# A feed-forward of two layers: plain products against Strassen's seven, through DRAM

## The chip, the cores and the metric

The kernel runs on one core of a Trainium2 chip. The metric is the device time of one execution in microseconds. A core has TensorE (PE in the profile; its weight loads are PEld), VectorE (DVE), ScalarE (ACT), GpSimd (POOL) and SyncE (SP, which here only issues DMAs), each with its own queue that runs in order. SBUF is the on-chip memory of 128 partitions; matmuls write PSUM, 8 banks of 512 fp32 columns.

## The reference

```python
def reference(q, k, v, moe_w_in, moe_w_out, moe2_w_in, moe2_w_out):
    # 4 batches, 8 heads, 576 tokens, head size 64; causal window of 128, a bias by distance
    scores = where(mask, q @ k.T / sqrt(64) + bias, -1e9)
    attn_out = softmax(scores) @ v
    x = attn_out.transpose(0, 2, 1, 3).reshape(2304, 512)
    h = x @ moe_w_in                               # 512 -> 2048
    x = (h * sigmoid(1.702 * h)) @ moe_w_out       # 2048 -> 512
    h = x @ moe2_w_in
    g = where(h >= 1, h, where(h <= -1, 0, (h + 1) ** 2 / 4))
    return g @ moe2_w_out
```

## The kernel before

Attention comes first (`attend` on each engine): 32 heads in 4 batches, 5 blocks of queries a head, software-pipelined by fixed lags. Its result stands transposed in `x_all` (features on partitions, all 2304 tokens).

Then two feed-forward layers, each over 6 chunks of 384 tokens (`feed_forward`, loops over chunks are hardware loops from chunk 1 on). To keep fp32 precision at one pass a column, each operand is split in two parts: `hi` is the value rounded to fp32r (ScalarE copies), `lo` is the value less `hi` (a VectorE subtraction), and a product is three matmuls: hi·hi, hi·lo, lo·hi. For each of 16 tiles j of 128 hidden features, `up` runs 12 matmuls of 384 columns (4 feature tiles x 3) into one of 4 PSUM banks. ScalarE applies the activation out of PSUM (layer 1: one Gelu_apprx_sigmoid; layer 2: `activate` with two Relu, `clip` on VectorE, `square` on ScalarE, a sum on VectorE), VectorE rounds and splits it (`split_activations`), and `down`, two tiles behind, adds it into 4 accumulator banks (layer 1: 4 x 3 matmuls of 384 columns, weights stationary, result transposed) or 3 (layer 2: 3 x 3 matmuls of 512 columns, activations stationary, result in rows of tokens). The 16 weight tiles of a layer (512 KB each) come by DMA through the ring `w_raw` of 3, are rounded and split once in the first chunk (`round_weights`, `split_weights`) and stay in SBUF. A chunk's result goes back into `x_all`, in layer 2 from there to `out`.

While attention ends, `FIRST_UPS` puts the first three `up` of 12 matmuls between its last steps on TensorE, and GpSimd splits the first three weight tiles and the first chunk of x.

All order is written out by hand: each engine's program text is its order, and semaphores tie the engines.

## Time and profile before

| | us |
|---|---|
| median of 3 runs | 973.02 (972.94 to 973.79) |
| the profiled execution | 972.23 |
| its span, first to last instruction | 970.4 |

| slices 1 to 40, tenths busy | |
|---|---|
| PE | 5999999999999999999999999999999999999998 |
| DVE | 6777774653213223232232277644444544544543 |
| ACT | 4777787332112121111121166543443533434433 |
| POOL | 3666574000000000000000000000000000000000 |
| DMA | 9966850430000000000000034010100100100101 |

The span is cut in 40 equal slices of 24 us; a digit is the busy share in tenths. Attention is the first 7 slices, layer 1 runs to slice 23, layer 2 to the end. A matmul's record overlaps the next one's, since matmuls are pipelined: their pace is read from starts, or from the chain, and not from the mean duration of one. The granted clock is 0.999 over the span.

### The profile page before, as it was taken

To read this page: it belongs to the slowest core of one execution; us is meant where nothing else is said; L and a number is where in the kernel's file an instruction comes from. 1 tells how busy PE (TensorE), PEld (TensorE's weight loads), DVE (VectorE), ACT (ScalarE), POOL (GpSimd) and SP (SyncE) were. 2 spreads that over 40 slices of the span, in tenths; PEclk is the share of its full clock that TensorE was granted. 3 is DMA by queue.
4 is the path that set the end of the run, shared out by engine and by line. 5 is a ranking of instruction groups with operands and counts; after the bars stand their busy time and mean duration, and the time that the engine had idled before them with its cause. 6 is when DMAs were issued, how large, how long until landed. Compare 5 with 4: busy or idle time off the path is not lost.

```text
span 970.4 us, 16335 instructions
## 1 busy us (share of the span) xinstructions
PE 955.9 (99%) x5584; PEld 903.1 (93%) x5584; DVE 443.4 (46%) x1156; ACT 377.9 (39%) x907; POOL 96.0 (10%) x71
## 2 busy tenths in 40 slices
PE   5999999999999999999999999999999999999998
PEld 5999999999999999999999999899999999998997
DVE  6777774653213223232232277644444544544543
ACT  4777787332112111121121166543443433534433
POOL 3666574000000000000000000000000000000000
PEclk9999999999999999999999999999999999999999
DMA  9966850430000000000000034010100100100101
GB/s 228 228 163 157 221 130 28 131 130 22 1 1 0 0 0 0 0 0 0 0 0 0 0 131 133 20 33 1 33 0 0 32 0 0 32 0 0 32 0 32
DMA packets 27729, 46.62 MB, mean 48 GB/s; under 512 B 5040, under 2 KB 19504, under 8 KB 27696
## 3 DMA queue, kind: packets, MB, share of 16 engines
q1 hardware_dynamic: 27696, 46.21, 18.0%
q8 instruction: 17, 0.28, 0.1%
q14 instruction: 16, 0.13, 0.1%
HBM read 41.48 MB, written 4.72 MB: 48 GB/s over the span
## 4 chain that ended last, share of the span: by engine, by line
PE 98%; DMA 1%; SPq 0%; DVE 0%; issue 0%; ACT 0%; DVEq 0%
PE bank L463 41%; PE bank L409 41%; PE bank L370 7%; PE bank L334 5%; PE bank L351 3%; PE bank L383 1%; DMA qk_raw<-qkT 1%; PE bank L390 0%; SPq L230 0%; DVE qk_hi L638 0%; DVE qk_hi L644 0%; ACT x_all L573 0%; SPq L258 0%; SPq L259 0%; DVE probs L657 0%
## 5 line engine op out<-in xcount | busy, mean ns | idle before, releaser
L586 ACT ACTIVATE act_a<-bank 128x384 f32<-128x384 f32 x96 | 47.1, 490 | 306.4 <-PE bank L409 306.4
L409 PE MATMUL bank<-x_hi,w_hi_b 128*128 128x384 f32 x480 | 161.6, 337 | 0.0
L409 PE MATMUL bank<-x_hi,w_lo_b 128*128 128x384 f32 x480 | 161.5, 336 | 0.0
L409 PE MATMUL bank<-x_lo,w_hi_b 128*128 128x384 f32 x480 | 161.3, 336 | 0.0
L713 DVE CAST g_hi<-act_a 128x384 fp32r<-128x384 f32 x96 | 34.5, 359 | 266.3 <-PE bank L463 251.0
L589 ACT ACTIVATE act_a<-bank,halves 128x384 f32<-128x384 f32 x96 | 55.6, 579 | 193.2 <-PE bank L409 193.2
L409 PE MATMUL bank<-x_hi,w_hi_a 128*128 128x384 f32 x288 | 97.2, 337 | 0.0
L409 PE MATMUL bank<-x_hi,w_lo_a 128*128 128x384 f32 x288 | 96.9, 336 | 0.0
L409 PE MATMUL bank<-x_lo,w_hi_a 128*128 128x384 f32 x288 | 96.8, 336 | 0.0
L409 PEld LDWEIGHTS bank<-x_hi,w_hi_b 128*128 128x128 f32 x480 | 90.2, 188 | 2.8
L409 PEld LDWEIGHTS bank<-x_lo,w_hi_b 128*128 128x128 f32 x480 | 90.3, 188 | 2.7
L409 PEld LDWEIGHTS bank<-x_hi,w_lo_b 128*128 128x128 f32 x480 | 90.3, 188 | 0.0
L753 DVE TENSOR_SCALAR act_a<-act_a 128x384 f32<-128x384 f32 x96 | 34.5, 360 | 118.4 <-ACT act_a L589 118.4
L708 DVE TENSOR_TENSOR act_r<-act_a,act_r 128x384 f32<-128x384 f32 x96 | 53.6, 558 | 63.4 <-ACT act_a L596 63.4
L463 PE MATMUL bank<-g_hi,w_lo_b 128*128 128x384 f32 x240 | 80.7, 336 | 0.0
L463 PE MATMUL bank<-g_lo,w_hi_b 128*128 128x384 f32 x240 | 80.7, 336 | 0.0
L463 PE MATMUL bank<-g_hi,w_hi_b 128*128 128x384 f32 x240 | 80.7, 336 | 0.0
L505 ACT ACTIVATE probs<-probs,neg_max 128x256 f32<-128x256 f32 (+2 forms) x160 | 74.3, 467 | 15.2 <-DVE neg_max L657 13.5
L370 PE MATMUL bank<-v_sb,probs_t 128*128 128x64 f32 (+2 forms) x576 | 76.0, 263 | 0.1
L370 PEld LDWEIGHTS bank<-v_sb,probs_t 128*128 128x128 f32 (+2 forms) x576 | 67.2, 178 | 5.7 <-issue 0.5
L463 PE MATMUL bank<-w_hi_b,g_lo 128*128 128x512 f32 x180 | 71.0, 394 | 0.0
L463 PE MATMUL bank<-w_lo_b,g_hi 128*128 128x512 f32 x180 | 70.9, 394 | 0.0
(75 smaller groups left out, 1856.4 us busy)
## 6 DMA issues: line engine op xcount, KB each, us to landing
qk_raw<-qkT SPq DMA_DIRECT2D x64, 288.0 KB, 4.6
w_raw<-w_tiles SPq DMA_DIRECT2D x32, 512.0 KB, 3.3
out<-x_all SPq DMA_DIRECT2D x18, 256.0 KB, 2.7
v_sb<-v_main SPq DMA_DIRECT2D x32, 128.0 KB, 4.1
bias_sb<-bias_table SPq DMA_DIRECT2D x8, 128.0 KB, 5.8
v_sb<-v_tail SPq DMA_DIRECT2D x32, 16.0 KB, 3.9
ident<-identity SPq DMA_DIRECT2D x1, 64.0 KB, 3.9
```

Source lines behind the costliest of these rows:

```text
L334: last = nc.tensor.matmul(score_bank[n % SCORE_RING][0:rows, 0:BAND], qk_hi[:, slot, 0, blk * P:blk * P + rows], k[:, key0:key0 + BAND], s ...
L351: last = nc.tensor.transpose(pt_bank[half][0:keys, col:col + rows], probs[0:rows, n % PROB_RING, piece * P:piece * P + keys], ident[0:rows ...
L370: last = nc.tensor.matmul(o_bank[0:rows, blk * DIM:(blk + 1) * DIM], probs_t[0:keys, half, col:col + rows], v_sb[0:keys, h, key_tile], sta ...
L383: last = nc.tensor.transpose(xt_bank[:, blk * P:(blk + 1) * P], heads_out[:, blk, pair * P:(pair + 1) * P], ident[:])
L409: last = nc.tensor.matmul(hid_bank[j % HID_RING][:, 0:CHUNK], w(j)[:, 0, k * P:(k + 1) * P], x[:, k], start=n_mm == 0, stop=n_mm == 3 * KT ...
L463: last = nc.tensor.matmul(to, stationary, moving, start=j == 0 and n_pass == 0, stop=j == FT - 1 and n_pass == 2)
L505: nc.scalar.activation(at, at, ACT.Exp, bias=neg_max[0:rows, n % PROB_RING:n % PROB_RING + 1], scale=-1.0, accum_out=sums[0:rows, h % SUM_ ...
L586: nc.scalar.activation(act_a[:, s], hidden, ACT.Gelu_apprx_sigmoid).then_inc(act_ready, 1)
L589: nc.scalar.activation(act_a[:, s], hidden, ACT.Relu, bias=halves[:, 0:1], scale=0.5).then_inc(act_first, 1)
L708: nc.vector.tensor_tensor(act_r[:, s], act_a[:, s], act_r[:, s], ALU.add).then_inc(act_summed, 1)
L713: nc.vector.tensor_copy(g_hi[:, s], g[:, s]).then_inc(g_rounded, 1)
L753: nc.vector.tensor_scalar(act_a[:, s], act_a[:, s], 1.0, None, ALU.min).then_inc(act_clipped, 1)
```

## The change

Strassen's algorithm multiplies two matrices, each cut in 2 x 2 quadrants, with 7 products of quadrants for 8 (in Winograd's form here). The left operand's sums are S1 = A21 + A22, S2 = S1 - A11, S3 = A11 - A21, S4 = A12 - S2; the weights get three chained sums for each tile (`add_weights`: 2 quadrants at once, 1, 1). The products are P1 (A11), P5 (S1), P6 (S2), P2 (A12), P7 (S3), P3 (S4), P4 (A22), in this order, and TensorE adds them in PSUM onto copies ("seeds") of partial sums: C11 = P1 + P2; P6 goes onto P1; C12, C21 and C22 are built from that with D1 = P5.

The work: 4 phases u (layer u // 2, half of the hidden features u % 2). A phase is up over 3 chunks of 768 tokens, then down over 3 chunks; these are the 8 phases of the title line, 4 up and 4 down. A chunk is two halves of 384 tokens by two halves of the features. A "duo" D is two hidden tiles in each half at once: an up chunk has two duos, a down chunk one. A product of a duo has two halves (`pos`), each of 6 matmuls of 384 columns in up, 12 of 384 in down of layer 1, and in down of layer 2 36 matmuls of 256 columns for both.

The other engines, for each chunk k and each duo D (all in the order of `up` and `down` on each queue):
- `round_operand` (ScalarE) and `split_operand` (VectorE) for each of the 7 operands, 768 columns in up and 1536 in down; `sum_operand` (VectorE) for S1 to S4.
- `seed_b` twice, `copy_d` twice, `seed_c` (ScalarE, out of PSUM; seeds also into PSUM); C11 and C21 by ScalarE, C22 and C12 by VectorE. In phases of odd u the down results are added to a partial result that is loaded back (`load_partial`, `add_c11`, `add_c21`).
- The activation: layer 1 Gelu_apprx_sigmoid on C11 and C21 out of PSUM and on 1536 columns in SBUF; layer 2 a clip to [-1, 1] of 3072 columns (VectorE), a square with bias and scale (ScalarE) and a maximum with g (VectorE), 3072 columns each.
- Weights: 8 tiles a phase of 512 KB, through one staging buffer `wst`, which is loaded again only when the tile before is split. In up, tiles w2 and w3 are prepared in chunk 0, w4 and w5 in chunk 1, w6 and w7 in chunk 2; w0 and w1 of the next phase in the first two down chunks.

Through DRAM go x (`store_pair`, `load_x`), the hidden activations (`store_hidden`, 1.57 MB a duo; `load_hidden`, four loads of 0.79 MB a down chunk) and the results of every phase (`store_y`). All are issued on SyncE's queue in one fixed order, each behind its waits. All loops of the feed-forward are unrolled. In attention, the pairs of heads go to `x_pairs` instead of `x_all`, and ScalarE, VectorE and GpSimd prepare two weight tiles and four operands in the last batch; `FIRST_PRODUCTS` puts three product halves (18 matmuls) and two marks between the last attention steps.

The core of the diff:

```diff
-CHUNK = 384
+HALF = 384
+CHUNK = 2 * HALF
...
+PHASES = 4
+DUOS = 9
+OPS = 7
+P1, P5, P6, P2, P7, P3, P4 = range(OPS)
+A11, S1, S2, A12, S3, S4, A22 = range(OPS)
...
+        def multiply(u, up, k, D, i, pos, bank, start):
+            at = operand(k, i)
+            dd = D % DUOS % 2
+            if up:
+                w = w_op(8 * u + 2 * dd + pos, i)
+                steps = [(bank, w[:, wh, kt * P:(kt + 1) * P], at[:, xh, kt])
+                         for kt in range(2) for wh, xh in ((0, 0), (0, 1), (1, 0))]
+            elif u < 2:
+                steps = [(bank, w_op(8 * u + 4 + kt, i)[:, wh, pos * P:(pos + 1) * P], at[:, xh, kt])
+                         for kt in range(4) for wh, xh in ((0, 0), (0, 1), (1, 0))]
+            else:
+                steps = [(bank[:, n * 2 * P:(n + 1) * 2 * P], at[:, xh, kt, (2 * pos + n) * P:(2 * pos + n + 1) * P],
+                          w_op(8 * u + 4 + kt, i)[:, wh])
+                         for n in range(2 - pos) for kt in range(4) for wh, xh in ((0, 0), (1, 0), (0, 1))]
...
+        def product_6(u, up, c, k, D, n):
+            pe.wait_ge(lo_made, OPS * k + S2 + 1)
+            pe.wait_ge(seeded_b, 2 * D + n + 1)
...
+        def product_4(u, up, c, k, D, n):
+            pe.wait_ge(lo_made, OPS * k + A22 + 1)
+            pe.wait_ge(c22_done, D + 1)
```

From ScalarE's `up`:

```diff
+        def up(u, c):
+            k = up_chunk(u, c)
+            D = up_duo(u, c, 0)
+            seed_b(D, 0)
+            round_operand(k, S3)
+            seed_b(D, 1)
+            round_operand(k, S4)
+            copy_d(D, 0)
+            if c:
+                activate(u, c - 1, 1)
+            if c == 0:
+                round_weights(8 * u + 2)
+            seed_c(D)
+            copy_d(D, 1)
+            round_operand(k, A22)
+            up_c11(u, c, 0)
+            if c == 0:
+                round_weights(8 * u + 3)
+            if c == 1:
+                round_weights(8 * u + 4)
+            up_c21(u, c, 0)
+            D = up_duo(u, c, 1)
+            seed_b(D, 0)
+            if c < 2:
+                round_operand(k + 1, A11)
+            seed_b(D, 1)
+            copy_d(D, 0)
+            activate(u, c, 0)
+            if c == 2:
+                round_weights(8 * u + 6)
+            seed_c(D)
+            copy_d(D, 1)
+            if c == 2:
+                round_operand(k + 1, A11)
+            round_operand(k + 1, S1)
+            up_c11(u, c, 1)
```

From VectorE's `up` (k is the up chunk, u the phase, c the chunk in it), and from SyncE:

```diff
+            sum_operand(k, S3)
+            sum_operand(k, S4)
+            if u >= 2 and c:
+                clip(u, c - 1, 1)
+            if c == 0:
+                add_all_weights(8 * u + 2)
+            split_operand(k, S3)
+            split_operand(k, S4)
+            if c == 0:
+                split_weights(8 * u + 2)
+            if u >= 2 and c:
+                larger(u, c - 1, 1)
+            split_operand(k, A22)
+            if c == 0:
+                add_all_weights(8 * u + 3)
+            if c == 1:
+                add_all_weights(8 * u + 4)
+            if c == 2:
+                add_all_weights(8 * u + 6)
+            up_c22(u, c, 0)
...
+            up_c12(u, c, 0)
+            if u >= 2:
+                clip(u, c, 0)
+            sum_operand(k + 1, S1)
+            if c == 2:
+                split_weights(8 * u + 6)
+            split_operand(k + 1, A11)
+            if u >= 2:
+                larger(u, c, 0)
+            split_operand(k + 1, S1)
+            sum_operand(k + 1, S2)
+            if c == 1:
+                add_all_weights(8 * u + 5)
+            if c == 2:
+                add_all_weights(8 * u + 7)
+            up_c22(u, c, 1)
...
+        def load_weights(w):
+            wait_past(sp, w_ready, 2 * w)
+            sp.dma_start(wst[:, 0:4], w_pairs[w]).then_inc(w_in, 16)
...
+            load_hidden(u, 1, 1, 1)
+            if u < 3:
+                load_weights(8 * u + 8)
+            store_hidden(u, 2, 1)
+            if u % 2:
+                load_partial(u, 0)
+            load_hidden(u, 1, 1, 0)
```

## Rows read from the trace of the kernel before

**Rows 1.** The page's first part: span, busy time and share of each engine

```profile
span 970.4 us, 16335 instructions
PE 955.9 (99%) x5584; PEld 903.1 (93%) x5584; DVE 443.4 (46%) x1156; ACT 377.9 (39%) x907; POOL 96.0 (10%) x71
```

**Rows 2.** The page's chain that ended last, by line

```profile
PE bank L463 41%; PE bank L409 41%; PE bank L370 7%; PE bank L334 5%; PE bank L351 3%; PE bank L383 1%; DMA qk_raw<-qkT 1%; PE bank L390 0%; SPq L230 0%; DVE qk_hi L638 0%; DVE qk_hi L644 0%; ACT x_all L573 0%; SPq L258 0%; SPq L259 0%; DVE probs L657 0%
```

**Rows 3.** TensorE's waits: line, waited for, us in total, times, longest

```profile
PE bank L334 <- DVE qk_hi L644: 8.3, 1, 8.3
...
PE bank L463 <- DVE x_all L686: 0.4, 1, 0.4
```

**Rows 4.** The chain in order of time: start us, us, what

```profile
299.21 6.24 PE bank L409 x36
...
692.74 6.29 PE bank L463 x27
```

**Rows 5.** Instructions in order of time (start, us): TensorE and weight loads, scores

```profile
120.05 0.28 PE L334 MATMUL bank<-k_lo,qk_hi 128*128 128x256 f32 x1
120.16 0.27 PE L351 MATMUL bank<-ident,probs 128*128 128x128 f32 x1
...
119.36 0.19 PEld L334 LDWEIGHTS bank<-qk_hi 128*128 128x128 f32 x1
119.47 0.19 PEld L334 LDWEIGHTS bank<-k_lo,qk_hi 128*128 128x128 f32 x1
```

**Rows 6.** VectorE by line and form: count, busy us, mean ns of one, idle before

```profile
L715 DVE TENSOR_TENSOR g_lo<-act_a,g_hi 128x384 fp32r<-128x384 f32 x96 | 53.6, 559 | 3.3
L694 DVE TENSOR_TENSOR w_lo_b<-w_raw,w_hi_b 128x1024 fp32r<-128x1024 f32 x20 | 24.4, 1218 | 0.0
L753 DVE TENSOR_SCALAR act_a<-act_a 128x384 f32<-128x384 f32 x96 | 34.5, 360 | 118.4 <-ACT act_a L589 118.4
```

**Rows 7.** ScalarE by line and form, same columns

```profile
L543 ACT ACTIVATE x_hi<-x_all 128x384 fp32r x40 | 17.6, 513 | 0.5
L531 ACT ACTIVATE w_hi_b<-w_raw 128x1024 fp32r<-128x1024 f32 x20 | 21.0, 1052 | 0.5 <-DMA w_raw<-w_tiles 0.5
L586 ACT ACTIVATE act_a<-bank 128x384 f32<-128x384 f32 x96 | 47.1, 490 | 306.4 <-PE bank L409 306.4
```

**Rows 8.** Order of time: instructions back to back, and behind another engine

```profile
578.18 1.22 DVE L694 TENSOR_TENSOR w_lo_a<-w_raw,w_hi_a 128x1024 fp32r<-128x1024 f32 x1
579.32 0.35 DVE L753 TENSOR_SCALAR act_a<-act_a 128x384 f32<-128x384 f32 x1
...
238.56 0.34 PE L409 MATMUL bank<-x_hi,w_lo_a 128*128 128x384 f32 x1
238.93 0.49 ACT L586 ACTIVATE act_a<-bank 128x384 f32<-128x384 f32 x1 [1.59 <-PE bank L409]
...
701.22 0.58 ACT L589 ACTIVATE act_a<-bank,halves 128x384 f32<-128x384 f32 x1 [1.48 <-PE bank L409]
701.70 0.58 ACT L590 ACTIVATE act_r<-bank,halves 128x384 f32<-128x384 f32 x1
701.83 0.36 DVE L753 TENSOR_SCALAR act_a<-act_a 128x384 f32<-128x384 f32 x1 [2.66 <-ACT act_a L589]
```

**Rows 9.** Busy time by stretch (last: clock, DMA share, GB/s); landings of w_raw

```profile
555.00:590.00 35.00, 35.00 (x189) 33.11 (x188) 25.10 (x43) 22.15 (x37) 0.00 (x0) 1.00 0.36 121
...
DMA to landing us min/median/max: 3.1/3.3/6.6
```

**Rows 10.** Order of time: TensorE after its first wait

```profile
9.03 0.41 PE L334 MATMUL bank<-k_lo,qk_hi 128*128 128x256 f32 x1
9.24 0.41 PE L334 MATMUL bank<-qk_hi 128*64 128x256 f32 x1
...
14.92 0.41 PE L334 MATMUL bank<-k_lo,qk_hi 128*64 128x256 f32 x1
...
16.30 0.28 PE L334 MATMUL bank<-k_lo,qk_hi 128*128 128x256 f32 x1
```

More of the change, by code:

```diff
@@ L489, in chunk @@
-    def chunk(c, k=None):
-        return x_all[:, k, bass.ds(c * CHUNK, CHUNK)]
+        for u in range(PHASES):
+            for c in range(CHUNKS):
+                for dd in range(2):
+                    duo(u, True, c, up_chunk(u, c), up_duo(u, c, dd))
+            for c in range(CHUNKS):
+                duo(u, False, c, down_chunk(u, c), down_duo(u, c))
     @block.scalar
@@ new lines, in y_free, with down_c11 @@
+        def y_free(engine, u, c):
+            wait_past(engine, y_stored, 16 * (u * CHUNKS + c))
+        def down_c11(u, c):
+            D = down_duo(u, c)
+            act.wait_ge(p2_done, D + 1)
+            y_free(act, u, c)
+            if u == 2 and c == 0:
+                act.wait_ge(g_ready, 2 * CHUNKS * (u + 1))
+            if swapped(D):
+                for pos in range(2):
+                    last = nc.scalar.activation(y_rows((0, 0), pos), by_block(b_bank(D, pos)), ACT.Copy)
+            else:
+                last = nc.scalar.activation(y_tile((0, 0)), b_both(), ACT.Copy)
+            last.then_inc(c11_out, 1)
@@ L624, in _ @@
+        for u in range(PHASES):
+            for c in range(CHUNKS):
+                up(u, c)
+            for c in range(CHUNKS):
+                down(u, c)
     @block.vector
@@ new lines, in down_c12 @@
+        def down_c12(u, c):
+            D = down_duo(u, c)
+            dve.wait_ge(p3_done, D + 1)
+            if swapped(D):
+                for pos in range(2):
+                    other = y_rows((0, 1), pos) if u % 2 else by_block(d1(D, pos))
+                    last = nc.vector.tensor_tensor(y_rows((0, 1), pos), by_block(c_bank(D, pos)), other, ALU.add)
+            else:
+                other = y_tile((0, 1)) if u % 2 else d1_both(D)
+                last = nc.vector.tensor_tensor(y_tile((0, 1)), c_both(), other, ALU.add)
+            last.then_inc(c12_done, 1)
@@ new lines, in add_c11 @@
+        def add_c11(u, c):
+            D = down_duo(u, c)
+            dve.wait_ge(p2_done, D + 1)
+            dve.wait_ge(y_loaded, 16 * (u // 2 * CHUNKS + c + 1))
+            if swapped(D):
+                for pos in range(2):
+                    last = nc.vector.tensor_tensor(y_rows((0, 0), pos), by_block(b_bank(D, pos)), y_rows((0, 0), pos), ALU.add)
+            else:
+                last = nc.vector.tensor_tensor(y_tile((0, 0)), b_both(), y_tile((0, 0)), ALU.add)
+            last.then_inc(c11_out, 1)
@@ new lines, in add_c21 @@
+        def add_c21(u, c):
+            D = down_duo(u, c)
+            dve.wait_ge(p4_done, D + 1)
+            if swapped(D):
+                for pos in range(2):
+                    last = nc.vector.tensor_tensor(y_rows((1, 0), pos), by_block(a_bank(D, pos)), y_rows((1, 0), pos), ALU.add)
+            else:
+                for part in a_parts(D):
+                    last = nc.vector.tensor_tensor(y_tile((1, 0))[:, part], a_part(D, part), y_tile((1, 0))[:, part],
+                                                   ALU.add)
+            last.then_inc(c21_out, 1)
@@ L781, in build @@
+        for u in range(PHASES):
+            for c in range(CHUNKS):
+                up(u, c)
+            for c in range(CHUNKS):
+                down(u, c)
     ctx.close()
```

1060 lines of the change are left out of this document (748 added, 312 removed).

## The prediction

> **What bounds the kernel now.** I read the page's first part, then the chain that ended last, then TensorE's waits. TensorE holds 955.9 of 970.4 us [rows 1]; the chain is TensorE nearly throughout, 41% of the span in each of the two feed-forward lines [rows 2]; it waits 8.3 us at the very start and 0.4 us at the hand-over to the feed-forward [rows 3]. So from 172 us on it streams without a wait: a matmul less is time less, unless a wait takes its place. The next busiest engines are at 46% and 39% [rows 1], but these are averages over a span in which they idle most of the time, and the change gives them nearly all of its added work. Whether they stay hidden is the whole question.
>
> **The matmuls.** The chain gives the pace: 36 of 384 columns in 6.24 us, 173.3 ns each; 27 of 512 columns in 6.29 us, 233.0 ns [rows 4]. Before: 2304 (up) + 1152 (down, layer 1) = 3456 of the first kind, 599 us, and 864 of the second, 201 us: 800 us. After, a duo of up has 7 products x 2 halves x 6 = 84 of 384 columns; 24 duos are 2016. Down of layer 1: 7 x 2 x 12 = 168 in each of 6 chunks, 1008. Down of layer 2: 7 x 36 = 252 of 256 columns in 6 chunks, 1512. The 256-column form stands in the scores only: the next record starts 0.11 us after one [rows 5], half of the 512 form is 116.5 ns; bounds 110 and 120, I take 116.5. After: 3024 x 173.3 = 524 us and 1512 x 116.5 = 176 us, 700 us. The four marks of 512 columns add 0.9. The span without new waits is 970.4 - 800 + 700 + 0.9 = 871 us (bounds 861 and 877).
>
> The 384 and 512 rows cost more per matmul than the Trainium skill has it (TensorE: Matmul & The Clock Gate, Back-to-back issue gap: columns / 2.4 + 2.5 ns, thus 162.5 and 216 ns). By that rule, an estimate, the saving would be 92 us and not 100. The trace disagrees, and I go by it.
>
> **What the other engines get, per instruction.** VectorE: a tensor_tensor of 384 columns is 558 ns, of 1024 columns 1218 ns, 1.03 ns a column; a tensor_scalar of 384 is 360 [rows 6]. ScalarE: 513 and 1052 ns out of SBUF, 490 for 384 out of PSUM [rows 7]. Back to back the next record starts before the last ends, 0.08 us early on VectorE and 0.10 on ScalarE [rows 8], so an instruction takes its engine T = 0.87 us (768 columns), 1.66 (1536), 3.25 (3072) on VectorE, and 0.73, 1.38 out of SBUF and 0.39 (384), 0.71 (768) out of PSUM on ScalarE. ScalarE writing PSUM (the seeds) is in no row: at most like the PSUM read, at best nothing to it but the columns, 0.32; I take 0.39. The clip of 3072 columns is by 384's rate between 1.7 (its fixed part paid once) and 2.9; I take 1.7. The square, 3072 columns at ScalarE's rate, is 2.7. From TensorE's last column to ScalarE 0.2 us, between ScalarE and VectorE 0.13 us after the engine is free [rows 8]. A weight tile takes 1.5 (three sums) + 2.0 (two splits) on VectorE and 1.7 on ScalarE.
>
> VectorE in an up chunk (29.2 us of matmuls): 11 sums and splits 9.6, four result sums 3.5, two weight tiles 7.0: 20.1 us; in layer 2 two clips and two maxima more, 9.9: 30.0 us. There VectorE is over TensorE even without one wait. In the third chunk of a phase the next operands are double size, 4.0 more. A down chunk has 20 to 27 us on VectorE. ScalarE has 18 to 22 us in each. Averages fit in layer 1; what costs is the order, since each product waits for a sum, a rounding and a split.
>
> **The walk.** I went through one up phase of each layer, counting from the start of P1 of a duo (slot 1.04 us: P7 is due at 8.3, P3 at 10.4, P4 at 12.5). P4 waits for C22, which VectorE makes after P7.
> - Chunk 0, first duo. The down chunk before leaves VectorE two splits behind; S3 is summed at 4.4, ScalarE's second seed stands behind its rounding and comes at 5.7, P6's second half was due at 4.2: 1.6 us. The second weight tile of the phase can be loaded only when the first is split (10.3; one staging buffer); it lands 3.3 us later [rows 9], is summed by 15.3, and C22 stands behind that sum: 16.2, 2.1 us late. Together 3.8 us, 4.3 in phase 0.
> - Chunk 1 to 2. The last split of tile w5 ends 3.5 us into chunk 2, S3 and the seed behind it: 1.7 us in layer 1. In layer 2 clip and maximum stand ahead too: 2.6 us in chunk 1, 4.5 in the first duo of chunk 2.
> - Chunk 2, second duo, the worst. VectorE reaches the split of w6 at 0.7, but ScalarE rounds w6 behind two seeds (2.7), the first copy of D1 (P5's half ends at 3.1; 3.7) and the activation of 1536 columns (5.1): rounded at 6.8. So the split ends at 8.6; A11 of the down chunk is rounded at 9.3 (seed C and the second copy of D1 go first) and split at 11.1, S1 split 12.7, S2 summed 14.4, w7 summed 15.9, C22 16.8. P4 was due at 12.5: 4.5 us with the handoff. In layer 2 the square (2.7 for 1.4) stands ahead of w6's rounding and the maximum (3.25) and the wait for A11 on VectorE: w6 split 9.9, A11 12.4, maximum 15.6, S1 17.3, S2 19.0, w7 20.5, C22 21.4: 9.0 us, and 0.5 for seed C. The first down product waits for w7's split, 0.3 to 0.5 us.
> - Down. First chunk: in phase 1 the partial sums stand ahead of C22, 1.9 us; in phase 2 seed C waits on ScalarE for w8 behind the maximum, 4; in phase 3 the stored hidden tile, the partial result and the next hidden tile (3.9 MB) follow the last maximum on the queue, at 336 GB/s (121 at a share of 0.36, [rows 9]) 12 us: 8 us. Phase 1's other two: 3.7; phase 3's: 1.
> - C21 of the duo before holds P1's second half, 0.1 us in 24 duos.
> Sums: phase 0 12, phase 1 16, phase 2 25, phase 3 31: 84 us. The bounds: without the ordering effects, only VectorE's surplus and the exposed loads, about 35; with clips at 2.9 and handoffs twice as long, 125.
>
> **The clock.** After the first wait of 8.3 us matmuls of 256 columns start 0.21 us apart (1.2 GHz), and records of 0.41 us still stand at 14.9 us, of 0.28 at 16.3 [rows 10]: about 7.6 us at half pace, 3.8 lost. The waits of 4.5 and 9 us are of that kind, though VectorE is late anyway behind them: I take 2 us at four places, 8 in all. (The Trainium skill, TensorE: Matmul & The Clock Gate, Why this matters for your kernels, warns of idle gaps of TensorE between bursts, that bring the half clock back; no row of this kernel has a gap in the feed-forward to show it.)
>
> The hand-over from attention costs nothing new: before, down starts at 172.1 behind 6.3 us of early up work; after, the chain pair tail, S3, rounding, seed gives P6's second half at about 171.5, behind 4.2 us of it. Cover is lost (18 filler matmuls for 36); were it gone entirely it would be 3 us. x stored and reloaded, 9.4 MB, goes beside attention, where DMA is at 0.6 to 0.98 share: nothing, at worst 5.
>
> Sum: 871 + 84 + 8 = 963 us of span; the profiled run lies 1.8 us over its span (972.2) and the median 0.8 over that: 966 us, 0.7% faster.
>
> **Rivals.**
> 1. Slower: the round trip through DRAM. Feed-forward traffic goes from about 20 MB to about 139 MB (24 hidden tiles of 1.57 MB, 38 out and 38 in; x 19; results 19 out and 9 back; weights 16), 175 GB/s, half of what the engines moved at full share. If landings double (the slowest weight tile before took 6.6 us against 3.3 [rows 9]): the second tile in four phases 13, x for the next phase in three last down chunks 16, hidden tiles in the first down chunks 12, w7 3: 45 us, 1011. A fifth of that doubling already carries it over the line. For: bursts of 1.6 MB; one queue that waits in order. Against: mean share about 0.5, large rows.
> 2. Slower: the half clock in every phase. If the 12 or so waits of over 1.5 us each cost the 3.8 us of the start, 46 for my 8: 1004. (The Trainium skill's rule above speaks for it.) Against: between these waits TensorE is at work.
> 3. Faster: the queues catch up where I have them late (seeds cheaper, VectorE's lag absorbed), waits 45: 925.
> 4. The 256-column form doesn't get its pace. A weight load's record is 0.19 us long; were it the pace, 1512 x 72 ns = 108 us more. Loads start 0.11 us apart in the scores [rows 5], which excludes nearly all.
>
> **How the numbers follow.** Forecast (948 to 985) 0.47; rival 1 0.17; rival 2 0.14; rival 3 0.20; rival 4 0.02. The line is at 973 less or more 1.9, the 0.2% that a measurement of this kernel can tell from no change. Of the forecast 0.32 lie below 971 and 0.05 within the line; mild forms of rivals 1 and 2 give 0.02 and 0.01. Faster 0.32 + 0.20 + 0.02 = 0.54; same 0.06; slower 0.40. The range leaves out the lower part of rival 3 and the upper of 1, 2 and 4: 928 to 1010.
>
> **What would show it.** Right: TensorE at about 90% of the span, waits for VectorE's C22 (P4) first, longest in the second duo of each third chunk and about twice as long in phases 2 and 3; the three up and three down chunks of a phase at 175 us without waits; 256-column matmuls 0.117 apart. Wrong: waits for DMA ahead of C22 (rival 1), half-clock stretches summing to over 30 us (rival 2), waits under 50 us in all (rival 3), attention ending later than before.

## The result, and the profile after

The changed kernel takes 1007.0 us (median of 4 runs, 1004.9 to 1008.2) against 973.2 (972.9 to 973.8): ratio 1.034, interval 1.0325 to 1.0363. It is 3.4% slower where the forecast was 0.7% faster. The profiled execution took 1004.9 us, its span is 1003.1, the granted clock 0.964 over it.

The page's first part and its slices (a slice is 25 us now), which answer to [rows 1] and to the table of slices of before:

```profile
span 1003.1 us, 16206 instructions
PE 902.9 (90%) x5804; PEld 869.9 (87%) x5804; DVE 711.7 (71%) x1061; ACT 548.1 (55%) x946; POOL 98.3 (10%) x70
...
PE   5999988799989998998989989877899899867997
...
DVE  5777776556569756666679679878786688786783
...
PEclk9999998999989999999989999997999999979899
```

TensorE has 100 us less in its matmuls, but its busy time fell by 53 only: by 60 in the feed-forward, where the records at half clock and those around a wait are longer, and in attention it rose by 7. What it lost beyond that is idle. VectorE went from 46% to 71%. The chain that ended last was TensorE nearly throughout [rows 2]; it now leaves it for 43% of the span:

```profile
PE 57%; DVE 24%; DMA 6%; ACT 6%; issue 6%; SPq 1%; POOL 0%; DVEq 0%; ACTq 0%; POOLq 0%
```

TensorE's waits, against the two of [rows 3] (line, waited for, us in total, times, longest). L731 is the matmul of `multiply`, L1266 C22 of an up duo, L949 `seed_b`, L1311 and L1315 C22 of a down chunk:

```profile
PE ps L731 <- DVE g L1266: 45.5, 16, 8.3
PE ps L731 <- ACT ps L949: 9.8, 8, 1.6
PE ps L731 <- DVE ust L1311: 9.2, 2, 8.2
PE ps L656 <- DVE qk_hi L1132: 8.7, 1, 8.7
PE ps L731 <- DVE ust L1315: 5.9, 3, 3.1
PE ps L692 <- DVE heads_out L1161: 3.4, 2, 3.0
```

P4's wait for C22 leads. The last row, a wait in attention, is new too, and I had not reckoned with it. From the starts of the weight loads, one ahead of each matmul of the seven products (each interval less its pace; over 0.6 us it is called a wait), the spans add up like this:

| us | before | forecast | after |
|---|---|---|---|
| up to the first feed-forward product | 162.2 | 162.2 | 176.4 |
| matmuls at their pace | 800 | 700 | 700.2 |
| waits in the feed-forward | 0 | 84 | 84.5 (33 of them) |
| half clock in the feed-forward | 0 | 8 | 17.2 |
| small losses at full clock | | (in the pace) | 11.2 |
| attention's last steps and marks between the products | 4 | 5 | 6.2 |
| behind the last matmul | 4.2 | 4.2 | 7.6 |
| span | 970.4 | 963 | 1003.1 |

The sum does not hang on the choice of starts, but the rows do: by the starts of the matmuls' own records the waits are 78 us (30 of them) and the small losses 17. So single waits are good to a few tenths, their sum to some 6 us.

### The profile page after: what moved, and what is told of

Same layout as the page of the kernel before. It is cut to its first block, busy times and chain, and to the rows that moved or that the text cites. A ratio compares the mean times of both kernels' runs of the same rounds, so it can differ in the third digit from the quotient of the medians.

```text
span 1003.1 us, 16206 instructions
## 1 busy us (share of the span) xinstructions
PE 902.9 (90%) x5804; PEld 869.9 (87%) x5804; DVE 711.7 (71%) x1061; ACT 548.1 (55%) x946; POOL 98.3 (10%) x70
## 4 chain that ended last, share of the span: by engine, by line
PE 57%; DVE 24%; DMA 6%; ACT 6%; issue 6%; SPq 1%; POOL 0%; DVEq 0%; ACTq 0%; POOLq 0%
PE ps L731 43%; DVE arena L1258 6%; PE ps L692 6%; PE ps L656 4%; DVE g L1287 4%; PE ps L673 3%; ACT ust L1000 2%; ACT arena L919 2%; DMA raw_rest<-gd 2%; DMA wst<-w_pairs 2%; DVE wst L1181 1%; DVE g L1266 1%; DVE raw_first L1243 1%; DVE w_first L1198 1%; DVE raw_first L1252 1%
## 5 line engine op out<-in xcount | busy, mean ns | idle before, releaser
L731 PE MATMUL ps<-arena,w_first 128*128 128x384 f32 x1764 | 347.6, 344 | 51.3 <-DVE g L1266 35.7
L731 PEld LDWEIGHTS ps<-arena,w_first 128*128 128x128 f32 x1764 | 317.2, 192 | 61.8 <-issue 59.2
L731 PE MATMUL ps<-arena,w_rest 128*128 128x384 f32 x1260 | 251.6, 344 | 13.7 <-DVE g L1266 9.7
L731 PEld LDWEIGHTS ps<-arena,w_rest 128*128 128x128 f32 x1260 | 225.6, 193 | 19.6 <-issue 19.0
L1258 DVE TENSOR_TENSOR arena<-raw_first,arena 128x768 fp32r<-128x768 f32 (+1 forms) x116 | 150.5, 1312 | 107.0 <-ACT arena L919 106.9
L919 ACT ACTIVATE arena<-raw_first 128x768 fp32r<-128x768 f32 (+1 forms) x120 | 131.9, 1117 | 93.2 <-DVE raw_first L1243 43.8
L731 PE MATMUL ps<-w_rest,arena 128*128 128x256 f32 x945 | 134.4, 284 | 8.2 <-DVE ust L1311 8.2
L731 PEld LDWEIGHTS ps<-w_rest,arena 128*128 128x128 f32 x945 | 123.1, 192 | 8.4 <-issue 8.4
L731 PE MATMUL ps<-w_first,arena 128*128 128x256 f32 x567 | 89.5, 285 | 3.0 <-ACT ps L965 2.0
L919 ACT ACTIVATE arena<-raw_rest 128x1536 fp32r<-128x1536 f32 (+1 forms) x48 | 61.0, 1271 | 40.5 <-DMA raw_rest<-gd 29.2
L1258 DVE TENSOR_TENSOR arena<-raw_rest,arena 128x1536 fp32r<-128x1536 f32 (+1 forms) x48 | 71.3, 1485 | 16.0 <-ACT arena L919 16.0
L692 PE MATMUL ps<-v_sb,probs_t 128*128 128x64 f32 (+2 forms) x576 | 78.1, 268 | 3.4 <-DVE heads_out L1161 3.4
L731 PEld LDWEIGHTS ps<-w_first,arena 128*128 128x128 f32 x567 | 77.8, 193 | 3.3 <-issue 3.3
L656 PE MATMUL ps<-qk_hi 128*128 128x256 f32 (+1 forms) x160 | 59.7, 376 | 10.4 <-DVE qk_hi L1132 8.7
L1287 DVE TENSOR_TENSOR g<-g,ust 128x3072 f32<-128x3072 f32 x12 | 40.3, 3356 | 13.6 <-ACT ust L1000 13.6
```

The lines of the kernel that those rows point to most:

```text
L656: last = nc.tensor.matmul(score_bank[n % SCORE_RING][0:rows, 0:BAND], qk_hi[:, slot, 0, blk * P:blk * P + rows], k[:, key0:key0 + BAND], s ...
L692: last = nc.tensor.matmul(o_bank[0:rows, blk * DIM:(blk + 1) * DIM], probs_t[0:keys, half, col:col + rows], v_sb[0:keys, h, key_tile], sta ...
L731: last = nc.tensor.matmul(to, stationary, moving, start=start and n == 0, stop=n == len(steps) - 1, skip_group_check=True)
L919: nc.scalar.activation(operand(k, i)[:, 0], source(k, i), ACT.Copy).then_inc(hi_made, 1)
L1258: nc.vector.tensor_tensor(at[:, 1], source(k, i), f32(at[:, 0]), ALU.subtract).then_inc(lo_made, 1)
L1287: nc.vector.tensor_tensor(g[:, e % 2], g[:, e % 2], ust[:], ALU.max).then_inc(g_ready, 1)
```

## Experiments

They ran in three groups, each beside the kernel before (its medians there: 973.4 for the first four that were put on record, 974.1 for the next four, 973.9 for the last two). "The changed kernel" is the one of the result, at 1007.0 us, and each edit is made to it unless another is named. In the cuts of code calls are shortened and "..." stands for what is left out.

**The order in the third chunk.** VectorE's and ScalarE's work in the second duo of each third up chunk, other order, nothing left out:

```diff
 ScalarE, second duo, c == 2
+            if c == 2:
+                round_weights(8 * u + 6)
             seed_b(D, 0)
...
             activate(u, c, 0)
-            if c == 2:
-                round_weights(8 * u + 6)
 VectorE, c == 2
             sum_operand(k + 1, S1)
             split_weights(8 * u + 6)
-            split_operand(k + 1, A11)
             if u >= 2: larger(u, c, 0)
-            split_operand(k + 1, S1)
-            sum_operand(k + 1, S2)
             add_all_weights(8 * u + 7)
+            split_operand(k + 1, A11)
             up_c22(u, c, 1)
-            up_c12(u, c, 1)
             split_weights(8 * u + 7)
+            split_operand(k + 1, S1)
+            sum_operand(k + 1, S2)
+            up_c12(u, c, 1)
```

> The second duo of each third up chunk waited 4.8, 4.9, 9.5 and 9.5 us for C22. Theory of the order: VectorE is idle for ScalarE's late rounding of w6 and has four things ahead of C22 that are not due yet. Here w6 is rounded first in the duo, and C22 goes ahead of S1's split and S2's sum. C22 then waits only for A11's rounding: these four waits fall to about 0.2, 0.2, 1.8 and 1.8 us, 24 us less in all, and the half-clock stretches behind them go (about 5 us more): 978 us (974 to 984). Rival, VectorE's load: with the engine full in layer 2, what is taken out of this place comes back at the next (first down product, C22 of the first down chunk): the two layer-1 waits go, the layer-2 ones move, 992 to 997 us.

984.9 us (982.1 to 987.7), ratio 1.011 (1.0089 to 1.013): 22 us of the 34 come back. In the changed kernel, this is the chain in the place in phase 2 (start us, us, what):

```profile
667.69 1.38 ACT w_rest L910
...
670.18 1.38 ACT arena L919
...
671.58 1.76 DVE arena L1258
673.34 3.27 DVE g L1287
676.61 1.68 DVE arena L1258
...
678.38 1.76 DVE raw_first L1243
680.14 0.61 DVE wst L1181
...
681.58 0.96 DVE g L1266
...
682.68 0.66 PE ps L731
```

w6 is rounded (L910), A11 of the down chunk rounded (L919) and split (L1258), then come the maximum (L1287), S1's split, S2's sum (L1243), the sums of w7 and at last C22, just in the order of the walk. TensorE, in order of time (bracket: idle before, and what ended it), first the changed kernel, then the reordered one:

```profile
669.91 4.43 PE L731 MATMUL ps<-arena,w_first 128*128 128x384 f32 x24 [0.60 <-ACT ps L968]
682.68 4.18 PE L731 MATMUL ps<-arena,w_first 128*128 128x384 f32 x12 [8.33 <-DVE g L1266]
```

```profile
671.91 2.32 PE L731 MATMUL ps<-arena,w_first 128*128 128x384 f32 x12 [1.51 <-DVE g L1266]
```

The wait of 8.3 us became 1.5, and the 12 matmuls behind it take 2.3 us and not 4.2. Over the four phases the waits of this duo were 4.8, 4.9, 9.5, 9.5 and are 0, 0, 1.8, 1.8: 25 us less. Of these 8 came back in the first down chunks (0, 3.4, 3.5, 8.4 became 1.3, 5.7, 5.2, 11.5). That is the rival at work in part: in phases 1 and 3 the chain into that C22 begins with the landing of a hidden tile (10.4 and 12.1 us), and that moved up by less than TensorE did. 984.9 is 1 us over the range of the order theory and 7 below its rival: the order was the cause of the largest waits.

**Part of the results loaded later.** The load of the partial result goes behind the first hidden tile of the chunk:

```diff
             store_hidden(u, 2, 1)
+            load_hidden(u, 1, 1, 0)
             if u % 2:
                 load_partial(u, 0)
-            load_hidden(u, 1, 1, 0)
```

> On SyncE's queue the partial result of the first down chunk in phases 1 and 3 is loaded behind the first quadrant of the next hidden tile (0.79 MB) instead of ahead of it. Theory: the sum S1 stands ahead of C22 on VectorE and waits for that quadrant, so the wait of 8.4 us in phase 3's first down chunk falls to about 5 (the partial, 1.57 MB, needs 4.7 us of the engines and is needed 2 us behind S1), and phase 1's 3.4 to about 2: 1002 us. Rival: both transfers are needed before C22 anyway and their sum sets the time: no change, 1007.

1000.5 us (998.9 to 1001.9), ratio 1.0284 (1.0266 to 1.0302). The first down chunk's wait went from 3.4 to 1.2 in phase 1 and from 8.4 to 6.1 in phase 3; phase 1's second lost 1.5 of it. So the queue's order counts, at about 2 us in each of the two. What is left of the wait in phase 3 is a load's again: the chain into that C22 now runs through the partial result, 11.66 us from issue to landing behind the store of the hidden tile (in the changed kernel it ran through the hidden tile, 11.96):

```profile
908.01 11.66 DMA ust<-zd
```

**The order of the down chunks.** On SyncE the next hidden tiles go ahead of the partial result and the store, on ScalarE and VectorE the next phase's weight tile behind the operands and C22 of the chunk:

```diff
-            store_hidden(u, 2, 1)
-            if u % 2:
-                load_partial(u, 0)
             load_hidden(u, 1, 1, 0)
             load_hidden(u, 1, 0, 0)
+            if u % 2:
+                load_partial(u, 0)
+            store_hidden(u, 2, 1)
             load_hidden(u, 1, 0, 1)
...
 VectorE's down
-            if weights:
-                add_all_weights(8 * u + 8 + c)
             split_operand(k, S4)
...
             down_c22(u, c)
+            if weights:
+                add_all_weights(8 * u + 8 + c)
```

> Down chunks alone: seed C, D1's copy, S4 and A22 go ahead of the next phase's weight tile on ScalarE, C22 ahead of its sums on VectorE, and on SyncE's queue the first two quadrants of the next hidden tile and the partial result go ahead of the store of the last hidden tile. My walk put 3.4, 3.5 and 8.4 us of waits in the first down chunks of phases 1, 2 and 3 on those three queues. Theory of the order: they fall to under 1, under 1 and about 1 to 2, the two half-clock stretches behind them go (7.5 us lost there), phase 1's other chunks stay at 3.4: 12 us of waits and 5 of clock, 990 us. Rival, DMA rate: the 3.9 MB must land anyway before the adds, so phase 3 keeps 4 or more: 997 us.

1002.0 us (997.4 to 1003.0), ratio 1.0262 (1.0223 to 1.03): 12 us over the theory and 5 over its rival. The three first chunks lost 11.7 us of wait (3.4, 3.5, 8.4 to 0.7, 0.0, 2.9), but the other two of phase 1 went from 0.9 and 2.5 to 4.0 and 6.3, with 4.1 us of half clock behind them. In phase 3 this edit moves nothing but SyncE's queue, since no weight tile is left to prepare: there the order of the transfers alone brought 8.4 down to 2.9. In phase 1 the chain shows who is late now: the partial result of the next chunk, and behind it the hidden tile (start us, us, what).

```profile
490.93 10.04 DMA ust<-yd
...
515.08 8.77 DMA yd<-ust
...
524.34 8.09 DMA raw_rest<-gd
```

So the expectation was nearly right at its place, and the gain was given back at the next: the buffer `ust` of the results is single, and store, load and sums go through it in a row. That no second buffer was tried leaves this last step argued.

**Attention's part moved.** This edit goes at two blocks in the queues at once, ScalarE's wait for x and VectorE's long split. In the last batch A11 and S1 are rounded later (steps 13 and 20 of 40, before 8 and 12), S2 and A12 after the last exponential, GpSimd's share a head later, and VectorE's split of each of the two weight tiles goes in four pieces between the steps:

```diff
-                    if n in (8, 12, 32, 36):
-                        round_operand(0, (A11, S1, S2, A12)[(8, 12, 32, 36).index(n)])
+                    if n in (13, 20):
+                        round_operand(0, (A11, S1)[(13, 20).index(n)])
...
-                    if n == 31:
-                        split_weights(1)
+                    if n in (31, 32, 33, 34):
+                        split_piece(1, n - 31)
```

> The feed-forward's first product started 14 us later than before. Theory: two blocks in the queues of the last batch do it. ScalarE's rounding of A11 waited for the load of x with the exponentials behind it (2.7 us), and VectorE's split of w1 (5 us beside GpSimd's subtractions) held the scores' bias and the head output, and behind each the clock fell. Here A11 and S1 are rounded five to eight units later, S2 and A12 after the last exponential, GpSimd's share moves one head later, and the six-operand splits of both tiles go in three pieces between other work. Expected: 10 to 12 us off, first product at about 165 us, 996 us; no half clock before it. Rival, plain load: attention has no room for this work with x's DMAs and the shared load of VectorE and GpSimd, wherever it stands: 3 us off at most, 1004.

1004.2 us (1002.4 to 1008.0), ratio 1.0311 (1.0294 to 1.0328), its interval overlapping the changed kernel's (1.0325 to 1.0363): the rival's outcome. In the changed kernel ScalarE stood for the load of x:

```profile
136.41 0.84 ACT L919 ACTIVATE arena<-raw_first 128x768 fp32r<-128x768 f32 x1 [2.72 <-DMA raw_first<-xd]
```

That wait is gone, and another stands in its place: VectorE's first sum of w1, with the score biases queued behind it.

```profile
146.27 0.69 DVE L1181 TENSOR_TENSOR wst<-wst 128x512 f32<-128x512 f32 x1 [7.58 <-DMA wst<-w_pairs]
```

The tile was asked for at 138.0 and took 8.2 us to land. The feed-forward starts at 176.7, as before the edit at 176.4.

**The second tile asked for earlier.** The same kernel, and w1's load goes right behind that of x instead of at the end of the batch:

```diff
             if q == 14:
                 load_x(0, 0)
+                load_weights(1)
-        load_weights(1)
```

> As e2_attention, and the load of the second weight tile goes out one pair of heads earlier on SyncE's queue (right behind the load of x). In e2 the wait moved: x was no longer waited for, but VectorE's sum of w1 stood 8 us of landing behind that load, with the scores' bias queued behind it, and attention ended as late as before. Theory, landings: attention's queues have room for the work, and only waits for late transfers break it. Expected: the feed-forward's first product at 166 to 168 us instead of 176.5, no half clock in front of it, 994 to 997 us. Rival, load: with x and w1 both there in time, attention still ends at over 173 us, since VectorE and GpSimd slow each other and ScalarE is full: 1002 to 1005 us.

1000.7 us (997.4 to 1003.4), ratio 1.0272 (1.024 to 1.0305); the feed-forward starts at 169.3, 7 us earlier, where I expected 166 to 168. With one of the two waits for loads in attention gone nothing was won, with both gone 7 us. The time itself lies between what I expected (994 to 997) and the rival's (1002 to 1005), and the spread of the runs covers most of that gap: half clock at 144.7 to 151.5 remains.

**Fills in the waits.** Matmuls of 384 columns into a bank that P4 does not read, ahead of P4 and behind the second copy of D1, extra work, nothing left out: 12 in each first duo of a phase; 24, 24, 50, 50 in the second duo of the third chunks; 16 and 44 in the first down chunks of phases 1 and 3:

```diff
             pe.wait_ge(lo_made, OPS * k + A22 + 1)
+            if D in fill:
+                pe.wait_ge(d_copied, 2 * D + 2)
+                for _ in range(fill[D]):
+                    nc.tensor.matmul(ps[:, 7, 0:HALF], ...)
             pe.wait_ge(c22_done, D + 1)
```

> Same kernel; in ten places where TensorE waits for C22 (12 matmuls in the first duo of each phase, 24 and 50 in the second duo of the third chunks, 16 and 44 in the first down chunks of phases 1 and 3) it runs matmuls whose result is thrown away, into the bank of P5, sized to end before the wait does. Theory of the clock: 17.2 us of the feed-forward are lost to the half clock behind such waits; without the gaps the granted clock stays up and 10 to 15 us go: 994 us. Rival, hidden: TensorE's slower pace falls in times in which VectorE is late anyway, so the records get faster and the next waits longer: 1003 to 1007 us. If the clock fell for another reason than the gaps, the half-clock stretches stay as they are.

997.2 us (994.4 to 998.6), ratio 1.0241 (1.0219 to 1.0262): the clock theory's outcome, 3 us over its 994 and 6 below the rival's 1003. The half clock in the feed-forward cost 4.6 us for 17.2, the granted clock is 0.986 over the span for 0.964. The place in phase 2 again; L805 are the fills, and the 12 matmuls behind them take 2.3 us:

```profile
672.42 8.83 PE L805 MATMUL ps<-arena,w_rest 128*128 128x384 f32 x50
681.09 2.27 PE L731 MATMUL ps<-arena,w_first 128*128 128x384 f32 x12
```

**Splits on GpSimd.** The two splits of w4 and w5 go from VectorE (whose surplus they are) to GpSimd, which idles in the feed-forward (the added lines are GpSimd's):

```diff
-            if c == 1:
-                split_weights(8 * u + 4)
+        for u in range(PHASES):
+            for w in (8 * u + 4, 8 * u + 5):
+                pool.wait_ge(w_rounded, 2 * w + 1)
+                nc.gpsimd.tensor_tensor(w_all(w)[:, 0, 1], wst[:, 0], f32(w_all(w)[:, 0, 0]), ALU.subtract)
...
```

> GpSimd, idle in the feed-forward, splits the two weight tiles of each second up chunk; VectorE loses 4 us of 88 in up in each phase. Theory of VectorE's load in layer 2: the waits of phases 2 and 3 in chunk 1 (1.1 and 2.0) and in the first duo of chunk 2 (4.4) come from its surplus, and go down by about 4 us a phase: 999 us. In layer 1 nothing changes. Rival, the engines slow each other: as in attention's last batch, where a VectorE subtraction of 1536 columns took 2.96 us beside GpSimd's against 1.75 alone, VectorE's work beside these takes as much longer as it is relieved: 1006 us or more.

1013.0 us (1012.1 to 1018.2), ratio 1.0392 (1.0362 to 1.0421): slower than the changed kernel, as the rival has it. VectorE and GpSimd in order of time:

```profile
232.12 3.51 POOL L651 TENSOR_TENSOR w_rest<-wst,w_rest 128x1536 fp32r<-128x1536 f32 x1 [1.88 <-ACT w_rest L919]
...
247.82 3.51 POOL L651 TENSOR_TENSOR w_rest<-wst,w_rest 128x1536 fp32r<-128x1536 f32 x1 [2.35 <-ACT w_rest L919]
```

```profile
232.47 0.96 DVE L1281 TENSOR_TENSOR g<-ps,d1s 128x768 f32<-128x768 f32 x1 [1.08 <-PE ps L740]
233.34 3.11 DVE L1247 TENSOR_TENSOR raw_first<-raw_first 128x768 f32<-128x768 f32 x1
...
248.50 3.64 DVE L1267 TENSOR_TENSOR arena<-raw_first,arena 128x768 fp32r<-128x768 f32 x1 [1.42 <-ACT arena L928]
```

A subtraction of 768 columns with both inputs in SBUF takes 0.96 us; one that starts while GpSimd's is under way ends 0.8 us after it (GpSimd's ends are 235.63 and 251.33, VectorE's 236.45 and 252.14). So it made next to no headway until GpSimd was done: a full stop, not a shared pace. The C12 sum at 232.47, one of whose inputs is PSUM, ran beside the same GpSimd instruction in its usual 0.96. The Trainium skill (SBUF — State Buffer, SBUF: two separate sides) says that a VectorE instruction with two SBUF inputs and a GpSimd instruction that reads SBUF share one pair of ports, which whichever starts first holds for its whole length; the trace agrees, for the sum that stopped (3.11) and for the one that did not (0.96).

**All reorderings together**, without the last two edits: third chunk, attention with the early tile, down order; besides, both seeds of the first duo ahead of S3's rounding, C22 of the first duo of a phase ahead of the sums of w3 (and C12 ahead of its split), and the last result stored in two halves (two lines of each of the first two):

```diff
 ScalarE's up
             seed_b(D, 0)
-            round_operand(k, S3)
             seed_b(D, 1)
+            round_operand(k, S3)
 VectorE's up
-            if c == 0:
-                add_all_weights(8 * u + 3)
             up_c22(u, c, 0)
+            if c == 0:
+                add_all_weights(8 * u + 3)
```

> All reorderings together: chunk 2's second duo (e1), attention's last batch with both transfers early (e5), the down chunks (e6), and three small ones: the second seed ahead of S3's rounding (8 waits of 1.6 us, of which C22's lateness gives back about half), C22 ahead of the sums of w3 in each chunk 0 (1.5 us in 4 places), the last result stored in two halves (2 us off the end). By the theory that orders and not loads cost the time: from 1007, e1's measured 22, e5's 11, e6's 17, these three 12, the clock's rest 3: 945 us, faster than the kernel before (973). If loads bound it, what is freed turns up elsewhere: 975 us.

969.8 us (964.9 to 971.4, 8 runs) against 974.1 (11 runs), ratio 0.994 (0.9917 to 0.9963): 0.6% faster than the kernel before, though 25 us over my expectation and 5 under the rival's. That expectation, on record before its parts had run, took 11 us for the attention edit and 17 for the down chunks, where alone they gave 6.3 and 5.0: 17 of the 25 us. The three measured gains, 22.1, 6.3 and 5.0, add up to 974, and the rest came from the small edits (behind the last product 5.5 us for 7.6, for one). 61.2 us of waits are left. In the first chunk of a phase w2 and w3 stand one behind the other in the chain, since both go through the one staging buffer (load, sums, rounding, split, and again; here in phase 0, start us, us, what):

```profile
181.09 3.58 DMA wst<-w_pairs
...
188.38 1.68 DVE w_first L1205
...
190.07 3.55 DMA wst<-w_pairs
...
195.29 1.49 ACT w_rest L915
...
196.81 1.77 DVE w_rest L1205
```

**The same with fills** in its remaining waits, fewer and shorter (12 in the first duo of a phase, 20 in two third chunks, 12, 24 and 24 in three down chunks):

```diff
+                    fill[up_duo(v, 0, 0)] = 12
+                fill[up_duo(2, 2, 0)] = fill[up_duo(3, 2, 0)] = 20
+                fill[down_duo(1, 1)] = 12
+                fill[down_duo(1, 2)] = 24
+                fill[down_duo(3, 0)] = 24
```

> e8_all with fill matmuls (384 columns, into a bank that P4 does not read) ahead of P4 in the waits that are left: 12 in the first duo of every first chunk, 20 in the first duo of the third chunk in phases 2 and 3, 12 and 24 in the second and third down chunk of phase 1, 24 in the first down chunk of phase 3. Clock theory: e8_all lost 13.3 us at half clock in the feed-forward; some 10 of them come back, 960 us, and the half-clock stretches after 190 us nearly all go. Rival: in e8_all the waits are shorter than in the changed kernel, and the fills of 3 to 4 us overshoot some of them: 966 to 970.

965.2 us (961.0 to 965.6), ratio 0.9899 (0.9876 to 0.9923). Half clock cost 4.5 us in the feed-forward for 13.3. The median lies between the theory's 960 and the rival's 966, and the intervals of the kernels with and without fills overlap a little; the clock shows the mechanism, while its price here is anything from nothing to some 8 us.

**GpSimd's splits out of VectorE's way in attention**, one thing more:

```diff
-            if h == 6:
-                split_done(h)
-                split_operand(S1)
             if h == 7:
                 split_done(h)
+                pool.wait_ge(w_ready, 4)
+                split_operand(S1)
```

> e9_all_filled with one thing more: GpSimd splits S1 only when VectorE has split w1 (the sum and the splits of S2 and A12 behind it follow), so no GpSimd operand work lies beside VectorE's split of w1. Contention theory: VectorE's pieces of that split take 0.42 to 0.67 us and not 1.5 to 2.0, the scores of heads 29 to 31 lose some 5 us less, the feed-forward starts at about 168 to 169 us and not 173.7, and the time is 4 to 5 us below e9_all_filled. Rival: VectorE's pieces are slow from the loads and stores of x in that stretch, not from GpSimd's splits, or the heads' own splits on GpSimd do the same: the pieces stay at 1.5 us or more, the start of the feed-forward moves by under 1 us, and S2, now later, may add 1 us.

963.8 us (963.0 to 964.6), ratio 0.9897 (0.988 to 0.9913): the same as without it. VectorE's pieces of w1's split (256, then three of 512 columns, of which the first and the last stand here; the middle one took 0.68 at 152.64) in this kernel:

```profile
147.03 2.04 DVE L1223 TENSOR_TENSOR w_first<-wst,w_first 128x256 fp32r<-128x256 f32 x1
...
150.90 1.48 DVE L1229 TENSOR_TENSOR w_first<-wst,w_first 128x512 fp32r<-128x512 f32 x1
...
153.59 0.68 DVE L1229 TENSOR_TENSOR w_first<-wst,w_first 128x512 fp32r<-128x512 f32 x1
```

and GpSimd in the same stretch (L619 splits A11, L603 and L606 split a head's q and k):

```profile
146.38 2.42 POOL L619 TENSOR_TENSOR arena<-raw_first,arena 128x768 fp32r<-128x768 f32 x1
148.87 1.47 POOL L603 TENSOR_TENSOR k_lo<-qk_raw,qk_hi 128x576 fp32r<-128x576 f32 x1
150.42 1.41 POOL L606 TENSOR_TENSOR qk_hi<-qk_raw,qk_hi 64x576 fp32r<-64x576 f32 x1
```

The two pieces with GpSimd idle take 0.68; the other two take 2.04 beside the split of A11, which the edit left where it was, and 1.48 beside a head's split, which every batch has. So the stop is real, as the theory has it, but the edit removed only part of it. Its price is not shown. In this profile the scores of head 25 start 1.9 us later than in the kernel with fills (full clock began at 20.7 us and not 18.0) and the feed-forward 2.4 earlier (170.5 for 172.8), 4.3 us gained between; but attention's program is the same in the three kernels before this one that have the tile early, and their profiles have the feed-forward start at 169.3 (the early tile alone), 173.7 (all reorderings) and 172.8 (with fills). 170.5 lies within that spread. In the time, 4 to 5 us were expected and 1.4 came, less than either interval. Whether a stop removed in attention is worth anything in the end is left open.

## Why the prediction was wrong, by its own steps

**The matmuls: right.** 3024 and 1512 of them at 173.3 and 116.5 ns are 700 us, and the span adds up with it. Rival 4 fell. But 11.2 us of small losses at full clock lie above it, 0.2 to 0.8 us in every duo, where I had 0.1 and the 256 form at its very pace. This is the first term that was mis-sized; its parts were not separated.

**The walk: right in its large places.** The waits come to 84.5 us where it had 84; that the sum fits so well is luck in part, since it moves by 6 us with the way of counting and misses of both signs cancel in it. Second duo of the third chunk: 4.8, 4.9, 9.5, 9.5 for 4.5, 4.5, 9.5, 9.5. First duo: 5.0, 4.2, 3.7, 5.1 for 4.3 and 3.8. First duo of the third chunk: 1.6, 1.7, 4.4, 4.4 for 1.7 and 4.5. First down chunks of phases 2 and 3: 3.5 and 8.4 for 4 and 8. Off were phase 1's down chunks, 3.4, 0.9, 2.5 for 1.9 and 3.7, and layer 2's second chunks, 3.2 and 3.1 for 2.6. The durations beneath it held as well: 768, 1536 and 3072 columns are 0.95, 1.75 and 3.36 us on VectorE before the overlap, the clip 1.76. That the order is the cause in the third chunks, and not the surplus of work, the reordered third chunk shows: same work, 22 us less.

**The clock: the mechanism right, half the size.** I had 2 us at four places, 8; it cost 17.2 in nine stretches of 3.4 to 10.2 us, 1.9 each. So the price of a place was right and their number wrong: taken singly, each of the eight longest waits (3.4 to 8.7 us) has such a stretch, one of the three next (2.5 to 2.9) has one, and none of the 22 shorter. This is what the stretch behind a wait of 8.3 us looks like in the columns of [rows 9] (length, busy time and count of PE, PEld, DVE, ACT and POOL, then clock, DMA share, GB/s), beside the one after it:

```profile
678.20:688.40 10.20, 5.72 (x21) 5.75 (x22) 7.02 (x9) 2.99 (x3) 0.00 (x0) 0.50 0.71 245
688.40:700.00 11.60, 11.60 (x101) 11.60 (x101) 10.89 (x7) 8.03 (x8) 0.00 (x0) 1.00 0.01 2
```

The slow stretch begins inside the wait and ends some 6 us after it. The step that failed is the count, "at four places": it took the third chunks only. It left out three first duos of a phase (single waits of 2.1 by the walk, 2.5 to 3.5 measured for the four) and two first down chunks, those of phases 1 and 3, though the walk had 8 us of wait for the second of them. The halved price rested on "VectorE is late anyway behind them", and the fills speak against that reason: they gave 10 us back, so the slow stretches were not hidden. Rival 2 had the effect of every wait at the 3.8 us of the start, 46 us; it is a third of that.

**The hand-over from attention: wrong, and the largest miss.** I had "costs nothing new" for the hand-over and "nothing, at worst 5" for x through DRAM; the feed-forward started 14.2 us later. The step that failed: for the last batch I priced TensorE's own chain and the transfers, these by DMA's mean share, and gave the work that ScalarE, VectorE and GpSimd get there no term at all, while its steps are in fixed order on every queue, as in the feed-forward, where I did walk. Against before, the scores start 1.8 us late from head 4 to 23 (full clock came at 19.4 us and not 15.9), 6.6 at head 27, 7.8 at 29, 13.8 at 30. The step to 6.6 is ScalarE's wait for x: its load took 8.9 us beside the stores and the next heads' loads, where [rows 9] had 3.3 for a third of the bytes; half clock from 138.9 to 142.3 follows it. The step to 13.8 falls where VectorE splits w1 beside GpSimd, in order of time,

```profile
149.78 2.04 DVE L1195 TENSOR_TENSOR w_first<-wst,w_first 128x256 fp32r<-128x256 f32 x1
151.74 2.96 DVE L1198 TENSOR_TENSOR w_first<-wst,w_first 128x1536 fp32r<-128x1536 f32 x1
...
155.11 0.55 DVE L1161 TENSOR_TENSOR heads_out<-ps,inverse 128x256 f32<-128x256 f32 x2
```

5 us in which no score gets its bias, where 2.1 were due (0.33 and 1.75 elsewhere), and TensorE then waits and falls to half clock from 155.9 to 162.8:

```profile
155.81 1.40 PE L692 MATMUL ps<-v_sb,probs_t 128*128 128x64 f32 x6 [2.98 <-DVE heads_out L1161]
```

Moving both gave nothing at first, since w1's load then stood in the way; with w1 asked for earlier it gave 7 us. How the 14.2 us divide between ScalarE's wait, VectorE's stop beside GpSimd and the clock behind each was not separated, and 7 of them stayed in the best case.

**The end: missed.** Behind the last matmul 7.6 us instead of 4.2. The last result leaves in one store, 5.7 us to landing, where the kernel before had 256 KB left to store, 2.7 us; I had counted no change. Stored in two halves, in the kernel with all reorderings, it was 5.5 us.

**Rivals.** Rival 1, the round trip: landings did grow, the medians (KB each, us to landing) are

```profile
raw_rest<-gd SPq DMA_DIRECT2D x32, 768.0 KB, 8.6
...
wst<-w_pairs SPq DMA_DIRECT2D x32, 512.0 KB, 3.5
```

but the weight tiles hardly (3.3 in [rows 9]). It did act in part. The waits for C22 in three down chunks (first and last of phase 1, first of phase 3: 3.4, 2.5 and 8.4 us) stood behind a landing in the chain, of a hidden tile, of x for phase 2 and of a hidden tile:

```profile
487.04 10.39 DMA raw_rest<-gd
...
559.29 6.31 DMA raw_first<-yd
...
911.52 11.96 DMA raw_rest<-gd
```

The walk had the last of them, at 8, and put phase 1's first, at 1.9, down to VectorE's sums. These are 14 us where rival 1 had 45 on top of the walk, so its 1011 us is near the measured 1007 by chance. Once C22's order is mended, loads are late in the down chunks of the reordered kernels too. Rival 3, queues that catch up, fell to the walk. Two of the prediction's own signs of being wrong came: the half-clock stretches sum to 58 us, over its 30, and attention ended later.

Sum of the misses: attention 14.2, clock 9.2, small losses 11.2, end 3.4, the rest 2: 40 us, on a forecast of 963 of span. With the rest as forecast, the attention miss alone makes 980 us, slower than before. The forecast lay 7 us below the kernel before, with three terms taken at nothing or near it, and each of them could only add time.

## What to carry to other kernels

Fewer matmuls are worth their time only as far as the operand work keeps up in its order. The walk of one period, instruction by instruction on every queue, found the largest waits, those of the third chunks, to within 0.4 us; attention, which I did not walk, came out 14 us late. So walk every stage that gets new work, the one that "has room" too. Price a wait of TensorE as the wait and what the clock loses behind it (here 17 us on 84), and where VectorE can't be made earlier, fill the wait with matmuls: that gave 10 us where the waits were long, and nothing certain where they were short. Expect gains of reorderings to be partly given back at the next late thing, 8 of 25 us here. Reordering alone brought the kernel from 3.4% slower to 0.6% faster, and with fills to 1.0% faster than before.

## What the runs showed of the hardware

- VectorE's subtraction with both inputs in SBUF stops for the whole of a GpSimd tensor_tensor that is under way: 0.96 us became 3.11 and 3.64 beside one of 3.51 (splits on GpSimd), 0.42 became 2.04 beside one of 2.4 (changed kernel). GpSimd waits the same way: its 1.41 became 2.80 beside VectorE's 2.96. A VectorE sum with one input in PSUM was not touched (0.96).
- A load of 1.57 MB took 8.9 us in attention (changed kernel) and one of 0.5 MB 8.2 (attention's part moved), where the median of that one over a whole kernel is 3.5.
- Half clock came in the feed-forward in nine stretches, 58 us together, 3.4 to 10.2 us each; with the waits filled three were left, 10 us together.
- ScalarE writing PSUM out of PSUM was no slower than writing SBUF out of PSUM: 476 ns for 384 columns (the seeds) against 483 (the copies of D1).
